# Two dense layers after routed experts: plain matmuls replaced by Strassen's seven products, in two phases with the activations kept in memory between them

## The reference, cut to what matters

```
h = x @ w_in              # x: 3072 x 512, w_in: 512 x 2048
r = np.maximum(h, 0.0)
g = r * r
return g @ w_out          # w_out: 2048 x 512
```

## Time and profile before

| | |
|---|---|
| time, median of 3 runs | 915.57 us (914.97 to 916.70) |
| the profiled execution, its span | 919.5 us |
| TensorE (PE) matmul busy | 902.2 us, 98% of the span, 5248 matmuls |
| VectorE (DVE) busy | 473.0 us, 51% |
| ScalarE (ACT) busy | 423.6 us, 46% |
| GpSimd (POOL) busy | 92.2 us, 10% |
| HBM read, written | 77.72 MB, 25.56 MB |

### The profile page before, as it was taken

How to read it: one execution, slowest core, us unless ns; L and a number is a source line. 1 busy time by engine, 2 the same in 40 slices (tenths; PEclk the granted TensorE clock), 3 DMA queues, 4 the chain that set the end, 5 groups by cost and what they waited for, 6 DMA issues and landing times.

```text
span 919.5 us, 17240 instructions
## 1 busy us (share of the span) xinstructions
PE 902.2 (98%) x5248; PEld 734.5 (80%) x5249; DVE 473.0 (51%) x1431; ACT 423.6 (46%) x978; POOL 92.2 (10%) x146
## 2 busy tenths in 40 slices
PE   9999999989899999999999999999999999999998
PEld 7878777767688887888888888888888888888886
DVE  5787899876566678763242224222422332243224
ACT  7888999855566668552232113211322221232123
POOL 3112222224222223100000000000000000000000
PEclk9999999999999999999999999999999999999999
DMA  5556775185677669740012003100400040004001
GB/s 200 172 166 201 234 230 172 69 302 199 222 251 248 224 220 357 260 96 0 1 52 41 1 0 75 17 0 0 91 0 0 0 91 0 0 0 91 0 0 46
DMA packets 87463, 99.55 MB, mean 108 GB/s; under 512 B 56189, under 2 KB 56317, under 8 KB 87408
## 3 DMA queue, kind: packets, MB, share of 16 engines
q1 hardware_dynamic: 81120, 83.07, 29.0%
q0 software_dynamic: 6000, 15.49, 4.9%
q10 hardware_dynamic: 288, 0.34, 0.1%
HBM read 77.72 MB, written 25.56 MB: 112 GB/s over the span
## 4 chain that ended last, share of the span: by engine, by line
PE 89%; issue 3%; DMA 3%; ACT 2%; DVE 2%; ACTq 1%; POOLq 1%; POOL 0%; DVEq 0%; SPq 0%
PE bank L1220 29%; PE bank L1193 28%; PE bank L1102 6%; PE bank L1083 6%; PE bank L930 4%; PE bank L985 4%; PE bank L958 4%; PE bank L996 1%; DMA routed<-pad_row 1%; PE bank L1091 1%; ACT prob L703 1%; PE bank L1010 1%; PE bank L978 1%; PE bank L1075 1%; DMA x_raw<-routed 1%
## 5 line engine op out<-in xcount | busy, mean ns | idle before, releaser
L1591 DVE TENSOR_TENSOR g<-relu_c 128x512 f32<-128x512 f32 x96 | 66.5, 693 | 340.1 <-ACT relu_c L873 340.1
L873 ACT ACTIVATE relu_c<-bank 128x512 f32<-128x512 f32 x96 | 57.5, 599 | 371.1 <-PE bank L1193 371.1
L1220 PE MATMUL bank<-w_hi,g_lo 128*128 128x512 f32 x384 | 150.1, 391 | 0.0
L1193 PE MATMUL bank<-x_hi,w_lo 128*128 128x512 f32 x384 | 149.6, 390 | 0.0
L1220 PE MATMUL bank<-w_hi,g_hi 128*128 128x512 f32 x384 | 149.4, 389 | 0.0
L1220 PE MATMUL bank<-w_lo,g_hi 128*128 128x512 f32 x384 | 149.4, 389 | 0.0
L1193 PE MATMUL bank<-x_hi,w_hi 128*128 128x512 f32 x384 | 149.4, 389 | 0.0
L1193 PE MATMUL bank<-x_lo,w_hi 128*128 128x512 f32 x384 | 146.5, 389 | 0.0
L703 ACT ACTIVATE prob<-score,neg_max 128x264 f32<-128x264 f32 (+1 forms) x192 | 94.0, 496 | 14.2 <-DVE neg_max L1283 14.1
L1546 DVE TENSOR_TENSOR w_lo<-w_raw,w_hi x70 | 82.0, 1221 | 10.5 <-ACT w_hi L816 7.1
L1220 PEld LDWEIGHTS bank<-w_hi,g_lo 128*128 128x128 f32 x384 | 72.1, 188 | 17.2 <-DVE g_lo L1598 2.5
(11 more groups left out here) (151 smaller groups left out, 1304.3 us busy)
## 6 DMA issues: line engine op xcount, KB each, us to landing
w_raw<-in_weights SPq DMA_DIRECT2D x80, 512.0 KB, 5.8
q_in<-in_qT SPq DMA_DIRECT2D x24, 256.0 KB, 3.3
v_in<-in_v SPq DMA_DIRECT2D x24, 256.0 KB, 3.6
x_rows<-x_row SPq DMA_DIRECT2D x24, 256.0 KB, 3.2
x_row<-x_rows SPq DMA_DIRECT2D x96, 64.0 KB, 2.5
k_in<-in_kT SPq DMA_DIRECT2D x23, 264.0 KB, 3.6
...
```

The source lines that it names most:

```text
L873: eng.activation(relu_c[:, f % 2, :], hc_ps[f % 2][:, :], ACT.Relu).then_inc(s_crelu, 1)
L1193: return eng.matmul(hc_ps[f % 2][:, :], w[f // UNIT][:, f % UNIT, wcols], x[:, c, :], start=begins, stop=ends)
L1220: ins = eng.matmul(yc_ps[s][:, :], gg[:, f % 2, s * P:(s + 1) * P], w[f // UNIT][:, f % UNIT, DM:CH], start=(f == 0 and n == 0), stop=(f = ...
L1591: eng.tensor_tensor(g[:, f % 2, :], relu_c[:, f % 2, :], relu_c[:, f % 2, :], ALU.mult).then_inc(s_cg, 1)
```

## The change

The dense layers use Strassen's scheme in the form with 7 products and 15 sums: a 2x2 block product is made of seven block products of sums of the blocks. Here a block of x^T is 256 features by 512 tokens, of w_in 256 by 256 columns of a quarter of the weights, and so on; tokens are taken 1024 at a time.

Phase one has 12 steps t (three groups of 1024 tokens by four quarters of w_in). A step makes the seven products in the order `PRODUCTS` (in step 0 `OPENING`), each with 12 matmuls of 512 columns into a pair of banks, in all 84. Their sums in PSUM and in q1 to q4 give four blocks of h: ScalarE copies product 1 to q1 (`p1_copy`) and makes relu and square of block 11 (`block11`); VectorE adds up the others (`u2`, `u3_z22`, `z21`, `z12`) and makes relu and square of each as one instruction (`relu_square`). Each block of g, 512 KB, is stored to `g_rows` in memory by SP, and q1 to q4 are written again only when the stores have landed. Products 2, 7 and 3 add onto banks that 1, 6 and 5 left, after these were read.

Phase two goes over the three groups; each has the seven products by four quarters of the hidden layer, 28 units of 12 matmuls. g comes back in 20 DMAs of 512 KB for a group; VectorE forms the sums (`t1` to `t4`, 16 for a group) and the lower part of each unit's operand (`unit_lower`), ScalarE the upper (`unit_upper`), in a ring of three. y is transposed back by VectorE (`turn_y`) and stored in pieces of 128 bytes.

The eight blocks that the weights' sums need are made on the chip: for the first two quarters of w_in by VectorE at the head of the last expert (`first_sums`), for the six other slices by GpSimd (`weight_sums`, four dependent or half dependent operations on 128x512), then split in three pieces each by ScalarE and VectorE (`slice_upper`, `slice_lower`) inside steps 1, 2, 9, 10 and 11 and behind step 11. A slice is 1 MB, loaded in two DMAs (`load_slice`). The x of groups one and two is loaded in steps 2 and 5, 32 DMAs each.

The core of the diff (the functions it takes out are printed above):

```diff
+FIRST = {1: 1, 2: 2, 4: 3, 5: 4, 6: 5, 7: 6, 3: 7}
+PRODUCTS = (1, 5, 6, 2, 7, 4, 3)
+LATER = {p: n + 1 for n, p in enumerate(PRODUCTS)}
+OPENING = (1, 2, 5, 6, 7, 4, 3)
+STEPS, QUARTERS, PIECES = 12, 4, ((1, 3), (3, 5), (5, 8))
...
+PAIR = {"a": (0, 1), "c": (4, 5), "b": (6, 7), "d": (2, 3)}
+pa, pc, pb, pd = (banks[:, n:m + 1, :] for n, m in PAIR.values())
+BANK_OF = {1: "a", 2: "a", 5: "c", 3: "c", 6: "b", 7: "b", 4: "d"}
...
+        elif f < HEAD:
+            eng.dma_start(w_raw[:, f, :], first_w[:, f, :]).then_inc(s_later[f], 16)
...
+    def load_slice(k):
+        eng.dma_start(w_in8[:, 0:2, :], later_w[k, :, 0:2, :]).then_inc(s_win, 16)
+        eng.dma_start(w_in8[:, 4:7:2, :], later_w[k, :, 2:4, :]).then_inc(s_win, 16)
+    def load_x(m, n, c, to, done):
+        first = m * BOTH + n * SUPER
+        rows = x_rows[first:first + SUPER, :].rearrange("(g t) (c b f) -> b t c g f", t=BLOCK, b=P // BLOCK, f=BLOCK)
         for b in range(P // BLOCK):
...
+            eng.dma_start(to[b * BLOCK:(b + 1) * BLOCK, :, :], rows[b, :, c, :, :]).then_inc(done, 16)
...
+    def store_g(t, blk, q, made, done):
+        eng.wait_ge(made, 2 * t + 2 if made is s_g11 else t + 1)
+        eng.dma_start(g_rows[t // QUARTERS, blk, t % QUARTERS, :, :], q[:, :, :].rearrange("p j t -> p (j t)")).then_inc(done, 16)
...
+    load_slice(0)
     eng.wait_ge(s_bscatter, tiles * 16 + 16)
     close(eng)
     eng.wait_ge(s_cturn, 4)
...
+    for c in range(DC):
+        load_x(0, 1, c, first_in[c], s_cx[c])
+    x_order = ((0, 0), (0, 1), (1, 0), (1, 1), (0, 2), (0, 3), (1, 2), (1, 3))
+    for t in range(STEPS):
+        if t in (2, 5):
+            if t == 2:
+                eng.wait_ge(s_wpl, 6)
+            else:
+                eng.wait_ge(s_xl, x_made(1, 3))
+            for n, (token_half, c) in enumerate(x_order):
+                load_x((t + 2) // 3, token_half, c, x_in[n], s_xin[n // 2])
+        if t == 9:
+            eng.wait_ge(s_xl, x_made(2, 3))
+            load_slice(2)
+        if t in (10, 11):
+            load_slice(t - 7)
+        if t == STEPS - 1:
+            for n in range(4):
+                eng.wait_ge((s_st11, s_st12, s_st21, s_st22)[n], 16 * QUARTERS)
+            load_chain(0, 0)
+            load_chain(0, 1)
+        store_g(t, B11, q4, s_g11, s_st11)
+        if t == 1:
+            eng.wait_ge(s_wpl, 3)
+            load_slice(1)
+        if t in (9, 10):
+            eng.wait_ge(s_wpl, 3 * (t - 6))
+        if t == STEPS - 1:
+            load_chain(0, 2)
+            load_chain(0, 3)
+            eng.wait_ge(s_wpl, 15)
+            load_slice(5)
+        store_g(t, B22, q3, s_g22, s_st22)
+        if t == STEPS - 1:
+            load_b12(0, 0)
+            load_b12(0, 1)
+        store_g(t, B21, q1, s_g21, s_st21)
+        if t == STEPS - 1:
+            load_b12(0, 2)
+            load_b12(0, 3)
+        store_g(t, B12, q2, s_g12, s_st12)
...
+    def weight_sums(k):
+        eng.wait_ge(s_win, 32 * k + 32)
+        a21, a11, s1, s2, a12, s3, a22, s4 = (w_in8[:, n, :] for n in range(8))
+        eng.tensor_tensor(s1, a21, a22, ALU.add).then_inc(s_wsum, 1)
+        eng.tensor_tensor(s3, a11, a21, ALU.subtract).then_inc(s_wsum, 1)
+        eng.wait_ge(s_wsum, 4 * k + 1)
+        eng.tensor_tensor(s2, s1, a11, ALU.subtract).then_inc(s_wsum, 1)
+        eng.wait_ge(s_wsum, 4 * k + 3)
+        eng.tensor_tensor(s4, a12, s2, ALU.subtract).then_inc(s_wsum, 1)
...
+    def slice_upper(k, piece):
+        first, end = PIECES[piece]
+        s = (k + 2) % 4
+        if k >= 2:
+            eng.wait_ge(s_one, halves(s + 8, 3 if k < 5 else (5, 2, 3)[piece]))
+        eng.wait_ge(s_wsum, 4 * k + 4)
+        eng.activation(w_hi[s // 2][:, first:end, s % 2 * SUPER:s % 2 * SUPER + SUPER], w_in8[:, first:end, :], ACT.Copy).then_inc(s_wph, 1)
...
+    def p1_copy(t):
+        eng.wait_ge(s_one, halves(t, 1))
+        wait(eng, s_st21, 16 * t)
+        eng.activation(q1[:, :, :], pa, ACT.Copy).then_inc(s_p1, 1)
+    def block11(t):
+        eng.wait_ge(s_one, halves(t, 2))
+        wait(eng, s_st11, 16 * t)
+        eng.activation(q4[:, :, :], pa, ACT.Relu).then_inc(s_g11, 1)
+        eng.wait_ge(s_g11, 2 * t + 1)
+        eng.activation(q4[:, :, :], q4[:, :, :], ACT.Square).then_inc(s_g11, 1)
...
+    def product(t, p):
+        m, s = t // QUARTERS, t % QUARTERS
+        w = operands(0, s, p)
+        if t == 0 and p == 1:
             eng.wait_ge(s_wlo, parts_ahead(E, tiles))
             close(eng)
...
+        if t in (2, 3):
+            eng.wait_ge(s_wpl, 3 * (t - 2) + (1, 1, 2, 2, 3, 3, 3)[LATER[p] - 1])
+        if s == 0:
+            eng.wait_ge(s_xh, x_made(m, p))
+        if t >= 1:
+            if p == 1:
+                eng.wait_ge(s_g11, 2 * t - 1)
+            elif p == 5:
+                eng.wait_ge(s_z12, t)
+            elif p == 6:
+                eng.wait_ge(s_u3, 2 * t)
+            elif p == 4:
+                eng.wait_ge(s_z21, t)
+        if p == 2:
+            eng.wait_ge(s_p1, t + 1)
+        elif p == 7:
+            eng.wait_ge(s_u2, t + 1)
+        for j in range(2):
+            if p == 3:
+                eng.wait_ge(s_z22, 2 * t + j + 1)
+            to = bank[PAIR[BANK_OF[p]][j]]
+            for c in range(2):
+                eng.matmul(to, w(w_lo, j, c), xh[p][:, c, :], start=(c == 0 and p in (1, 5, 6, 4)), stop=False, skip_group_check=True)
+                eng.matmul(to, w(w_hi, j, c), xh[p][:, c, :], start=False, stop=False, skip_group_check=True)
+            if s == 0 and j == 0:
+                eng.wait_ge(s_xl, x_made(m, p))
+            for c in range(2):
+                ins = eng.matmul(to, w(w_hi, j, c), xl[p][:, c, :], start=False, stop=(c == 1), skip_group_check=True)
+            ins.then_inc(s_one, 1)
...
+        hi, lo = ring_h[n % 3], ring_l[n % 3]
+        eng.wait_ge(s_th, n + 1)
+        for c in range(2):
+            for j in range(2):
+                eng.matmul(to[c], w(w_lo, j, c), hi[:, j, :], start=(q == 0 and j == 0 and p in (1, 5, 6, 4)), stop=False, skip_group_check=True)
+                eng.matmul(to[c], w(w_hi, j, c), hi[:, j, :], start=False, stop=False, skip_group_check=True)
+        eng.wait_ge(s_tl, n + 1)
+        for c in range(2):
+            for j in range(2):
+                ins = eng.matmul(to[c], w(w_hi, j, c), lo[:, j, :], start=False, stop=(q == 3 and j == 1), skip_group_check=True)
+        ins.then_inc(s_unit, 1)
...
+    for t in range(STEPS):
+        for p in order(t):
+            product(t, p)
+    for m in range(3):
+        for p in PRODUCTS:
+            for q in range(QUARTERS):
+                unit(m, p, q)
...
+    def first_sums():
+        eng.wait_ge(s_landed, UNIT * (E - 2) + HEAD)
+        a21, a11, a12, a22, s1, s2, s3, s4 = (w_raw[:, n, :] for n in range(8))
+        eng.tensor_tensor(s3, a11, a21, ALU.subtract).then_inc(s_wsums, 1)
+        eng.tensor_tensor(s1, a21, a22, ALU.add).then_inc(s_wsums, 1)
+        eng.wait_ge(s_wsums, 2)
+        eng.tensor_tensor(s2, s1, a11, ALU.subtract).then_inc(s_wsums, 1)
+        eng.wait_ge(s_wsums, 3)
...
+    def u2(t):
+        eng.wait_ge(s_one, halves(t, 6))
+        eng.wait_ge(s_p1, t + 1)
+        wait(eng, s_st12, 16 * t)
+        eng.tensor_tensor(q2[:, :, :], q1[:, :, :], pb, ALU.add).then_inc(s_u2, 1)
+    def u3_z22(t):
+        for j in range(2):
+            eng.wait_ge(s_one, halves(t, 7, j))
+            eng.tensor_tensor(q1[:, j, :], q1[:, j, :], bank[PAIR["b"][j]], ALU.add).then_inc(s_u3, 1)
+        for j in range(2):
+            if j == 0:
+                wait(eng, s_st22, 16 * t)
+            eng.wait_ge(s_u3, 2 * t + j + 1)
+            eng.tensor_tensor(q3[:, j, :], q1[:, j, :], bank[PAIR["c"][j]], ALU.add).then_inc(s_z22, 1)
+    def relu_square(q, ready, made):
+        eng.wait_ge(*ready)
+        eng.scalar_tensor_tensor(out=q[:, :, :], in0=q[:, :, :], scalar=0.0, in1=q[:, :, :], op0=ALU.max, op1=ALU.mult).then_inc(made, 1)
+    def z21(t):
+        eng.wait_ge(s_one, halves(t, 4))
+        eng.wait_ge(s_z22, 2 * t + 2)
+        eng.tensor_tensor(q1[:, :, :], q1[:, :, :], pd, ALU.subtract).then_inc(s_z21, 1)
+    def z12(t):
+        eng.wait_ge(s_one, halves(t, 3))
+        eng.wait_ge(s_u2, t + 1)
+        eng.tensor_tensor(q2[:, :, :], q2[:, :, :], pc, ALU.add).then_inc(s_z12, 1)
...
+    def t1(m, q):
+        eng.wait_ge(s_b12[q // 2], 32 * (m + 1))
+        eng.tensor_tensor(chain_g[q][:, :, :], b12_g[q][:, :, :], chain_g[q][:, :, :], ALU.subtract).then_inc(s_tsum, 1)
...
+    x_lower(0, 1, pb)
+    x_lower(0, 2, pd)
     for c in range(DC):
...
+        turn_first(c)
+    turned_to(2)
+    x_sum(chain_x, b12_x, pb)
+    x_lower(0, 5, chain_x)
+    turned_to(4)
+    x_sum(chain_x, b22_x, chain_x)
+    x_sum(b12_x, b22_x, b12_x)
+    x_lower(0, 6, chain_x)
+    x_sum(chain_x, chain_x, pd)
+    x_lower(0, 7, b12_x)
+    u2(0)
...
+    for t in range(1, STEPS):
+        m = t // QUARTERS
+        if t in (3, 6):
```

(46 more changed lines are left out.)

554 lines of the change are left out of this document (372 added, 182 removed).

## The result

The changed kernel takes 920.75 us (median of 4 runs, 919.8 to 921.18), the kernel before 915.66 (914.97 to 916.7): a ratio of 1.0061, with a 95% interval of 1.0048 to 1.0075. It is slower by 0.6%; 908.4, faster, was predicted, and the range held the time. The profiled execution has a span of 919.5 us and a granted clock of 0.972.

A forecast was written before the change was run, and what follows sets the result against it. TensorE was taken to bound the kernel: 67.3 us gained by fewer matmuls against 60.1 us of new gaps gave -7.2 us, so 915.57 became 908.4 us, with a range of 893 to 925.

The forecast's parts named there:

- phase two: Second phase of the new dense stage: VectorE busy 63 of 76.2 us a group, so no gap, 0 us.
- `first_sums` puts 4 sums of 512, 2.7 us: Last expert: VectorE's sums stand ahead of a block, so its lower part comes late for TensorE; 0.7 us lost.
- Steps 9 to 11: Phase one: late weight slices delay product 3, cycle 24.4 us instead of 19.04; 17.8 us lost, clock's part included.
- Steps 3 and 4: Phase one: stores behind 32 x loads in SP's queue delay `p1_copy`, then `z12` is late; 13.7 us lost.
- The joint: Between the phases: slice 5 is summed late, so the fourth and fifth units wait; 8.1 us lost.
- GpSimd's 1.28 us: GpSimd's sum on 128x512, for which no row existed: taken as 1.27 us, bounds 0.63 and 2.5.
- the end: Behind the last matmul: sum, two transposes, 8 issues and landing take 8.3 us against 4.1 before; 4.2 us lost.
- steps 6 and 8: Phase one: four transposes ahead of `z12` cost 1.7 us, then a lower part and a sum 0.9; 2.6 us lost.
- Step 0: Start of phase one: last scatter, 16 x loads and VectorE's list delay products 5 and 7; 13.0 us lost.
- Relu and square as one instruction save: VectorE in phase one: the fused form saves one instruction of 1.2 us a block, which no plain step waits for.
- The returns of the clock cost more, or each semaphore hop: Rival: clock returns dearer, or each hop in the long lists 0.1 more; 8 to 15 us, 916 to 923, chance 0.16.
- Dear GpSimd: Rival: sums at 2.5 us make slices 4.9 us later at four places; +19.8, 928 us, chance 0.13.

The follow-up runs named there:

- first_sums_out: Changed kernel without VectorE's four sums of 128x1024 for the first two quarters' weights, work left out; 916.9 us, ratio 1.0012.
- two_instructions: Changed kernel with relu and square of three blocks as a maximum and a product instead of one fused instruction; 938.27 us, ratio 1.0233.
- stores_between: Changed kernel with the 32 x loads of step 2 split among that step's four stores instead of all ahead of them; 923.25 us, ratio 1.0069.
- stores_and_list: Changed kernel with step 2's x loads split among its stores and, in VectorE's step 3, only two transposes ahead of `u2`; 913.62 us, ratio 0.9991.
- sums_twice: Changed kernel with GpSimd's four sums of slices 2 to 5 made twice each; 941.14 us, ratio 1.0291.
- the kernels with early slices: Changed kernel with slices 2 to 4 loaded as soon as their buffer is free, 897.16 us; the same with GpSimd's sums made twice, 918.46 us.

## Why the prediction was wrong

**The frame was right.** Fewer matmuls at an unchanged pitch against new gaps, nothing lost in phase two, each gap at the place and with the releaser that was named. The forecast lay on the wrong side since -7.2 us was the difference of 67.3 and 60.1, and the gaps measure 73.3. That the range held 920.75 is worth little: it was 32 us wide and had both signs in it.

**The steps that failed are terms of the sum that were sized too small.**
- "`first_sums` puts 4 sums of 512, 2.7 us": they are of 1024 columns, 4.8 us. That is a width misread in the diff. 0.7 became 4.5, of which the wait for `hb_lo` is 2.4 and the half clock behind it 1.6 (8 matmuls, 0.2 each); first_sums_out gives back 4.5.
- "Steps 9 to 11": "the cycle is 24.4", and it is 27.1. Product 3 was to start 20.7 us into the step and starts at 21.7, 22.1 and 21.8. The slice is two DMAs behind the store, and the second of them is issued 3.6, 4.4 and 3.6 us into the step, where the whole load was put at 2.7: their issue time on SP was left out. Landing (5.5 us after the last issue in step 10), sums (5.1) and split (5.2) are as worked out. From product 3's start to the step's end 3.7 us were to pass, and 0.9 for the clock; it takes 5.3, as all 12 matmuls of product 3 run at 1.2 GHz, and not 8. That is 1.1 and 0.7 us a step, 5.6 for three; the other 0.9 is that step 9 was given a shorter cycle than the two behind it, and has the same.
- "Steps 3 and 4": the 32 x loads keep SP's queue for 18.6 us (453.5 to 472.1), 0.58 each and not 0.53, one of them for 1.87. They were to be done 11.3 us into step 3 and are done at 13.1. Behind them q1's store lands after another 5.5 us, as forecast, so at 18.6 and not at 16.8, though the DMA engines are 95% busy from 470.5 to 478.5. 2.1 us; step 4 loses its 2.0 as forecast. Why some of the loads keep the queue longer is open.
- The joint: 1.2 us. The half clock behind step 11 was to be covered, but the fourth unit runs in it and takes 4.5 us instead of 2.7.

**What held.** GpSimd's 1.28 us, the x loads' 0.52 each in step 0, the end within 0.2, steps 6 and 8 within 0.5, phase two. Step 0 came within 0.7 us by errors that in part cancel. The scatter landed 2.7 us after its issue, not 3.9, and counted from that issue product 5 started 1.7 us earlier than forecast. But the half clock, which was to be covered by VectorE's work there too, makes products 5 and 6 late (granted clock 0.50 in 403.5 to 406.5), and VectorE waits for product 6 ahead of `u2`, which releases product 7. So product 7 came only 0.8 us earlier:

```profile
411.28 1.22 DVE L1919 TENSOR_TENSOR q<-q,banks 128x1024 f32<-128x1024 f32 x1 [1.07 <-PE banks L1483]
```

**Two claims that the experiments took away.** "Relu and square as one instruction save ... 1.2 us a block, which nothing waits for in a plain step": two_instructions loses 0.35 to 0.8 us in plain steps and up to 3.1 in others, for 0.7 us more a block. And step 3 can't be read from its releaser alone. In the changed kernel the store does decide: VectorE's transposes are done at 475.3, and it then waits 4.50 us for an upper part that stands behind `p1_copy` on ScalarE. But stores_between, which frees `p1_copy`, moves the loads back in the same queue, and VectorE's list ends where it did. The two edits of stores_and_list together win 6.4 us; the edit of VectorE's list alone was not run.

**The rivals.** "The returns of the clock cost more, or each semaphore hop", 916 to 923 at a chance of 0.16, is nearest to what came, though the clock has, as an estimate, 5 of the 13.2 us that were missing (2.2 in steps 9 to 11, 1.6 in the last expert, 1 at the joint). An issue without a price, a misread width and the longer x loads of step 2 have the rest. Dear GpSimd was wrong in its price, and sums_twice shows that the place was right: there 5.2 us more of sums for each of four slices cost 21 us. The Trainium skill (GPSIMD Engine Reference, section 8) says that GpSimd shares its SBUF interfaces with VectorE and contends with instructions that have two SBUF inputs. In the changed kernel's steps 9 to 11 this costs nothing, since VectorE stands still while GpSimd sums (its lower parts in step 10 start behind an idle stretch of 6.29 us). In the kernels with early slices the traces agree with it, as the last section tells.
